# A transformer-style kernel in which the softmax of an attention block is finished in the step that follows its selection, with sums and reciprocals on GpSimd

## The chip, the cores and the metric

The kernel runs on one core of one Trainium2 chip. The metric is the device time of one execution in microseconds; the median of three runs is taken.

## The reference

Three layers follow one another. The first is attention that keeps, in every row of scores, the 32 largest only (batch 4, 8 heads, 576 tokens, 64 numbers per head):

```python
scores = scale * np.matmul(q, k.transpose(0, 1, 3, 2))
kth = np.partition(scores, -top_k, axis=-1)[..., -top_k:-top_k + 1]
scores = np.where(scores >= kth, scores, -1000000000.0)
scores = scores - np.max(scores, axis=-1, keepdims=True)
attn = np.exp(scores)
attn = attn / (np.sum(attn, axis=-1, keepdims=True) + 1e-09)
x = np.matmul(attn, v)
```

The second is a dense layer over 2304 tokens of width 512: softplus(x @ w_in) @ w_out, with 2048 hidden numbers. The third sends each token to the best of 8 experts, relu(x @ w1[e]) @ w2[e] with 1024 hidden numbers, times its gate.

## The kernel before

**Blocks.** The attention is cut into 72 blocks (BLOCKS). A block has 128 rows of two heads, so its scores are two tiles t = 0, 1 of 128 x 576. Rows 0 to 511 of a batch give four row groups of four head pairs each; the last 64 rows of two batches are taken together in "ends" blocks.

**Steps.** Every engine runs its own program, written out by hand as a loop over steps i = -1 to 73 (TAIL = 74); semaphores join the five programs. There is no planner: the order of the calls in each engine's loop is the schedule. Block n is selected on VectorE while step n runs, masked and exponentiated in step n+1, and in step n+2 it is normalised, transposed and multiplied with v. From step 10 (MLP_AT) on each step also does an eighth of the dense layer for a group of 256 tokens (unit u of group g): "up" in step i, "down" of the unit before. Group 0 needs the attention of blocks 0 to 7. The operations, with their lines in the profile:

- TensorE: scores (L575, eight products, in "ends" blocks sixteen), which writes the banks that scores_out empties; turn_probs (L589 and L592, nine transposes), which waits for pr_ready of each half; times_v (L614, 20 products, in "ends" blocks 40), which waits for probs_out; up (L644 to L646, 24 products); down (L663 to L665, 12 products); in some steps the turning of tokens (L676) and the logits (L686). The scores of block i+3 are made in step i (scores_at, AHEAD = 3), at its start; in the first step of a group they stand amid "up", before the product that needs the last block's x.
- ScalarE: scores_out (L887, L890), cut_off (L898, the first half of a mask), exponentials (L905), normalise (L911), probs_out (L918), x_out (L924), rectify (L932, L933), logarithm (L938, L941), h_high (L949), split_wo (L955), split_wi (L961), down_out (L970).
- VectorE: the selection, in four rounds of eight maxima for each tile (maxima L1158, strike L1164); reciprocals (L1172 the sum of two numbers for the first blocks, L1175 the reciprocal).
- GpSimd: biases (L1502, L1504), x_split_up (L1512, L1514), denominators (L1521, the sum, from block 9 on), mask (L1529 after a cut_off; L1533 and L1536 without one, a longer form), softplus (L1541), h_low (L1547), low_wo (L1552), low_wi (L1558).
- SyncE's queue: the loads, and the stores of split pieces of w_out (L464), which are read back in every group (L472).

Weights are split into a high and a low part (split_wo, low_wo, split_wi, low_wi) in steps 1 to 10, a piece in each step. cuts(n) says which tiles of block n are masked with ScalarE's help: both before block FREE = 8, tile 0 only afterwards. The scores stand in a ring of five buffers; top in a ring of three; pr, bias, eps, den and rden in two buffers. After step 73 come the last group of the dense layer and then the experts, in an order of their own.

In a step from 10 on the order on ScalarE is

```python
h_high(i-1); x_out(i-3); cut_off(i-1); scores_out(i+3)
normalise(i-2, 0); normalise(i-2, 1); rectify(i)
probs_out(i-2); turn_out / logits_out; logarithm(i)
exponentials(i-1, 0); exponentials(i-1, 1); down_out
```

and on GpSimd x_split_up(i-3), h_low(i-1), mask(i-1), low_wi, softplus(i), biases(i), denominators(i-1). VectorE's reciprocals(n-2) stand in the second round of block n. Before step 10 they stand behind the selection of the next block, so block n is normalised once block n+1 is selected.

## Time and profile before

| | before |
|---|---|
| median of 3 runs | 1057.04 us (1056.1 to 1057.84) |
| profiled execution | 1057.04 us, of it 1054.8 us span |
| TensorE (PE) busy | 992.9 us, 94% |
| VectorE (DVE) busy | 817.3 us, 77% |
| ScalarE (ACT) busy | 727.6 us, 69% |
| GpSimd (POOL) busy | 711.9 us, 67% |
| chain that ended last | PE 80%, DVE 8%, POOL 4%, ACT 3% |

The profile is one execution. A busy TensorE is not one at its peak: its products overlap, and their ends are modelled. The shares are means over the span; the attention and dense layer together run to about 742 us, the experts after that, and there only TensorE is full. A row of the view in order of time has the start, the duration of the group (both in us), the engine, the line, the operation, what it writes and reads, how many, and in brackets the idle time before it with what ended it. PE are the products, PEld the weight loads.

### The profile page before, as it was taken

Reading aid. Unit: us, or ns where it says so; the run is one execution under the profiler, and the core shown is the slowest. Engines: PE = TensorE matmul, PEld = TensorE weight load, DVE = VectorE, ACT = ScalarE, POOL = GpSimd, SP = SyncE. Lnnn points to the kernel's source line nnn. Section 1 sums busy time; section 2 is a strip of 40 time slices with the busy share of each in tenths; the row PEclk is TensorE's granted clock in tenths of the full one; section 3 lists DMA queues with packets and bytes.
Section 4 is the critical chain, followed back from the end, with each engine's and each line's share of the span. In section 5 each row is a group of like instructions: output and inputs, shape, how many; then the busy total and the mean of one; then the engine's idle time right before and its main releaser. Section 6 shows DMA issues by size and latency. Waiting matters only on the chain.

```text
span 1054.8 us, 21596 instructions
## 1 busy us (share of the span) xinstructions
PE 992.9 (94%) x6878; PEld 806.3 (76%) x6879; DVE 817.3 (77%) x1744; ACT 727.6 (69%) x1390; POOL 711.9 (67%) x831
## 2 busy tenths in 40 slices
PE   5565899999999999999999999999999999999996
PEld 2343687788788788788788888887887788888875
DVE  7999999999999999999999999994345622222261
ACT  3888898988998998998888999998554111111140
POOL 2688898889899899899888899899351311111101
PEclk9996899999999999999999999999999999999999
DMA  9723253343344343324434333333481421111100
GB/s 311 257 91 127 112 171 121 128 143 121 114 153 165 114 157 121 124 98 144 169 119 155 117 120 102 121 121 121 156 331 54 165 96 52 40 40 40 40 20 20
DMA packets 43391, 130.99 MB, mean 124 GB/s; under 512 B 4320, under 2 KB 18656, under 8 KB 33056
## 3 DMA queue, kind: packets, MB, share of 16 engines
q1 hardware_dynamic: 40256, 120.09, 32.5%
q0 software_dynamic: 3040, 9.70, 2.7%
q8 instruction: 51, 0.84, 0.3%
q14 instruction: 44, 0.36, 0.1%
HBM read 111.95 MB, written 18.09 MB: 123 GB/s over the span
## 4 chain that ended last, share of the span: by engine, by line
PE 80%; DVE 8%; POOL 4%; ACT 3%; issue 3%; DMA 1%; SPq 1%; ACTq 0%; DVEq 0%; POOLq 0%
PE psum L614 8%; PE psum L575 7%; PE psum L644 7%; PE psum L737 6%; PE psum L739 6%; PE psum L738 6%; PE psum L646 6%; PE psum L645 6%; PE psum L663 6%; PE psum L665 6%; PE psum L664 6%; PE psum L589 5%; DVE top L1158 3%; DVE work L1164 3%; PE psum L769 2%
## 5 line engine op out<-in xcount | busy, mean ns | idle before, releaser
L1158 DVE MAX8 top<-work 128x8 f32<-128x576 f32 x432 | 305.4, 752 | 0.0
L1164 DVE MATCH_REPLACE8 work<-top,work 128x576 f32<-128x576 f32 x288 | 212.6, 749 | 0.0
L644 PE MATMUL psum<-x_parts,wi_hi 128*128 128x256 f32 x576 | 171.1, 297 | 0.0
L645 PE MATMUL psum<-x_parts,wi_hi 128*128 128x256 f32 x576 | 162.9, 283 | 0.0
L646 PE MATMUL psum<-x_parts,wi_lo 128*128 128x256 f32 x576 | 162.7, 283 | 0.0
L614 PE MATMUL psum<-prT,vtok 128*64 128x128 f32 (+3 forms) x1600 | 117.1, 287 | 15.2 <-ACT prT L918 15.2
L614 PEld LDWEIGHTS psum<-prT,vtok 128*64 128x64 f32 (+1 forms) x1600 | 85.5, 144 | 54.2 <-issue 41.2
L575 PE MATMUL psum<-kT,qT 64*128 64x512 f32 (+3 forms) x640 | 113.0, 480 | 11.5 <-DMA qT<-in_q 4.4
L1638 POOL DMA_INDIRECT out<-ys,dst_now x19 | 19.2, 1012 | 152.6 <-DVE ys L1360 150.7
L663 PE MATMUL psum<-wo_ring,h_hi 128*128 x288 | 119.1, 414 | 1.0 <-POOL h_lo L1547 0.9
L1541 POOL TENSOR_TENSOR hs<-hs,ab 128x512 f32<-128x512 f32 x72 | 93.7, 1301 | 32.7 <-ACT ab L941 32.5
L644 PEld LDWEIGHTS psum<-x_parts,wi_hi 128*128 128x128 f32 x576 | 109.9, 191 | 6.8 <-issue 2.4
L905 ACT ACTIVATE pr<-pr,bias 128x576 f32<-128x576 f32 x144 | 110.0, 766 | 6.7 <-POOL pr L1536 3.7
L665 PE MATMUL psum<-wo_ring,h_lo 128*128 x288 | 113.1, 393 | 0.0
L664 PE MATMUL psum<-wo_ring,h_hi 128*128 x288 | 112.7, 391 | 0.0
L645 PEld LDWEIGHTS psum<-x_parts,wi_hi 128*128 128x128 f32 x576 | 110.1, 191 | 0.2
L646 PEld LDWEIGHTS psum<-x_parts,wi_lo 128*128 128x128 f32 x576 | 110.1, 191 | 0.0
L911 ACT ACTIVATE pr<-pr,rden 128x576 f32<-128x576 f32 x144 | 104.4, 784 | 8.0 <-DVE rden L1175 8.0
L575 PEld LDWEIGHTS psum<-kT,qT 64*128 64x128 f32 (+1 forms) x640 | 57.5, 195 | 68.1 <-issue 59.4
L589 PE MATMUL psum<-ident,pr 128*128 128x128 f32 x576 | 81.3, 284 | 22.3 <-ACT sc L890 16.7
L1547 POOL TENSOR_TENSOR h_lo<-hs,h_hi 128x512 fp32r<-128x512 f32 x72 | 93.1, 1293 | 5.9 <-ACT h_hi L949 5.9
L589 PEld LDWEIGHTS psum<-ident,pr 128*128 128x128 f32 x576 | 66.6, 145 | 27.9 <-issue 17.6
(215 smaller groups left out, 2353.1 us busy)
## 6 DMA issues: line engine op xcount, KB each, us to landing
wo_ring<-wo_parts SPq DMA_DIRECT2D x72, 1024.0 KB, 4.8
wo_parts<-wo_ring SPq DMA_DIRECT2D x8, 1024.0 KB, 3.8
kT<-in_k SPq DMA_DIRECT2D x16, 288.0 KB, 3.4
qT<-in_q SPq DMA_DIRECT2D x16, 288.0 KB, 3.9
vtok<-in_v SPq DMA_DIRECT2D x16, 256.0 KB, 2.9
wo_raw<-in_moe_w_out SPq DMA_DIRECT2D x1, 4096.0 KB, 14.1
wi_raw<-in_moe_w_in SPq DMA_DIRECT2D x4, 1024.0 KB, 14.4
x_rows<-x2tok SPq DMA_DIRECT2D x16, 256.0 KB, 2.4
```

Of the source, the lines that this page charges most:

```text
L575: mm = nc.tensor.matmul(to[rows, :], qT[h * HD:(h + 1) * HD, p, cols], kT[h * HD:(h + 1) * HD, p, keys], start=True, stop=True)
L589: mm = nc.tensor.transpose(transit[:, j // 3, j % 3 * P:(j % 3 + 1) * P], pr_of(n)[:, first_key(t) + c * P:first_key(t) + (c + 1) * P], id ...
L614: mm = nc.tensor.matmul(x_raw_at[h * HD:(h + 1) * HD, cols], vtok[rows, p, c, h * HD:(h + 1) * HD], probs, start=(c == 0), stop=(c == FULL))
L644: nc.tensor.matmul(ps[:, part, :], wi_hi[:, u, kk, f], hi, start=first, stop=False)
L645: nc.tensor.matmul(ps[:, part, :], wi_hi[:, u, kk, f], lo, start=False, stop=False)
L646: mm = nc.tensor.matmul(ps[:, part, :], wi_lo[:, u, kk, f], hi, start=False, stop=last)
L663: nc.tensor.matmul(psum[:, 6 + a, :], high, hi, start=(f == 0), stop=False)
L664: nc.tensor.matmul(psum[:, 6 + a, :], high, lo, start=False, stop=False)
L665: mm = nc.tensor.matmul(psum[:, 6 + a, :], low, hi, start=False, stop=(f == KF - 1))
L905: nc.scalar.activation(pr[:, n % 2 * 2 + t, :], pr[:, n % 2 * 2 + t, :], ACT.Exp, bias=bias[:, n % 2, 0, t:t + 1], scale=1.0, accum_out=ep ...
L1158: nc.vector.max(top[:, at, 8 * r:8 * r + 8], sc_of(n)[:, t, :] if r == 0 else work[:, t, :]).then_inc(topk_step, 1)
L1164: nc.vector.match_replace(work[:, t, :], top[:, at, 8 * r - 8:8 * r], sc_of(n)[:, t, :] if r == 1 else work[:, t, :], TAKEN).then_inc(topk ...
```

## The change

- On ScalarE, GpSimd and TensorE the calls of a step stand in a new order. Before step 10 ScalarE does probs_out, cut_off, split_wo, the exponentials, x_out (now of block i-2), scores_out and then normalise of block i-1, the one exponentiated just before. TensorE turns and multiplies block i-2 ahead of the scores.
- From step 10 on ScalarE does the exponentials of block i-2 at the start of the step, with x_out between the two, then scores_out, h_high, normalise, rectify, probs_out, cut_off, logarithm. GpSimd does biases(i-1), mask(i-1), softplus(i), x_split_up(i-2), denominators(i-1), h_low(i).
- VectorE no longer computes sums and reciprocals; denominators on GpSimd does, for every block: the sum, then a power with exponent -1 of two numbers per partition.
- Scores are made two blocks ahead from step 10 on, and none in step 9. FREE is 9, so both tiles of block 8 are cut with ScalarE's help.
- The load of w_out is issued in two halves with a semaphore each, and split_wo waits for the half that it reads.

The diff:

```diff
--- before.py
+++ after.py
@@ -89,7 +89,7 @@
             LOGITS[up_step(g) + UNITS + 2 + 2 * a] = 2 * g + a
 
 
-    FREE = MLP_AT - 2
+    FREE = MLP_AT - 1
 
     def cuts(n):
         return (0, 1) if n < FREE else (0,)
@@ -153,6 +153,7 @@
         ident = sb("ident", [P, P])
         wg = sb("wg", [P, KD, E])
         slot_no = sb("slot_no", [P, 2], I32)
+        inverse = sb("inverse", [P, 2])
         lg = sb("lg", [P, NT, E])
         eps = sb("eps", [P, 2, 2, 2])
 
@@ -284,7 +285,8 @@
         dst_now = sb("dst_now", [P, 1], I32)
         slot_gate = sb("slot_gate", [P, COLS])
 
-        wi_loaded, wo_loaded, wg_loaded = sem("wi_loaded"), sem("wo_loaded"), sem("wg_loaded")
+        wi_loaded, wg_loaded = sem("wi_loaded"), sem("wg_loaded")
+        wo_loaded = [sem("wo_loaded_0"), sem("wo_loaded_1")]
         wi_hi_ready, wi_split = sem("wi_hi_ready"), sem("wi_split")
         wo_hi_ready, wo_split = sem("wo_hi_ready"), sem("wo_split")
         wo_stored = [sem("wo_stored_0"), sem("wo_stored_1")]
@@ -300,6 +302,7 @@
         xs_split, e_h_split = sem("xs_split"), sem("e_h_split")
         gathered = [sem(f"gathered_{i}") for i in range(XS)]
         ident_step, consts = sem("ident_step"), sem("consts")
+        inverse_ready = sem("inverse_ready")
         scores_ready, scores_copied = sem("scores_ready"), sem("scores_copied")
         half_block, ends_copied = sem("half_block"), sem("ends_copied")
         topk_step, mask_step, masked = sem("topk_step"), sem("mask_step"), sem("masked")
@@ -329,13 +332,17 @@
 
 
 
-        AHEAD = 3
+
+        RING = 5
 
         def scores_at(i):
-            return i + 1 if i <= 0 else i + AHEAD
+            return i + 1 if i <= 0 else i + 3 if i < MLP_AT - 1 else i + 2 if i >= MLP_AT else BLOCKS
+
+        def scores_made(i):
+            return min(i + 4, MLP_AT + 2) if i < MLP_AT else min(i + 3, BLOCKS)
 
         def sc_of(n):
-            m = n % (AHEAD + 2)
+            m = n % RING
             return sc[:, 2 * m:2 * m + 2, :] if m < 3 else sc_more[:, 2 * m - 6:2 * m - 4, :]
 
         def is_block(n):
@@ -453,7 +460,10 @@
                 load_qk(0, p)
             for p in range(PAIRS):
                 load_v(0, p)
-            sp.dma_start(wo_raw[:], w_out.rearrange("(k p) n -> p k n", p=P)).then_inc(wo_loaded, 16)
+            for half in range(2):
+                at = slice(half * KF // 2, (half + 1) * KF // 2)
+                sp.dma_start(wo_raw[:, at, :], w_out.rearrange("(k p) n -> p k n", p=P)[:, at, :]
+                             ).then_inc(wo_loaded[half], 16)
             for kk in range(KD):
                 sp.dma_start(wi_raw[:, :, kk, :], w_in[kk * P:(kk + 1) * P, :].rearrange(
                     "p (u f) -> p u f", u=UNITS)).then_inc(wi_loaded, 16)
@@ -577,11 +587,11 @@
                                                   start=True, stop=True)
                 mm.then_inc(scores_ready, 1)
 
-            def turn_probs(n):
+            def turn_probs(n, made):
                 if n:
                     pe.wait_ge(transit_copied, n)
                     pe.wait_ge(x_copied, n)
-                pe.wait_ge(scores_copied, 2 * min(scores_at(n + 2) + 1, BLOCKS))
+                pe.wait_ge(scores_copied, 2 * made)
                 for t in range(2):
                     pe.wait_ge(pr_ready, 2 * n + t + 1)
                     for c in range(FULL):
@@ -797,16 +807,26 @@
             for i in range(-1, TAIL):
                 late = is_block(i - 2)
                 n = scores_at(i)
+                if i < MLP_AT:
+                    if late:
+                        turn_probs(i - 2, scores_made(i - 1))
+                        times_v(i - 2)
+                    if is_block(n):
+                        scores(n, max(i - 1, 0))
+                    if i == 0:
+                        scores(n + 1, 0)
+                        scores(n + 2, 0)
+                    continue
 
                 amid = {}
                 if up_at(i) and up_at(i)[1] == 0 and is_block(n):
-                    amid[0, k_last(up_at(i)[0])] = lambda: scores(n, max(i - 2, 0))
+                    amid[0, k_last(up_at(i)[0])] = lambda: scores(n, i - 2)
                 elif is_block(n):
-                    scores(n, max(i - 2, 0))
+                    scores(n, i - 2)
                 if up_at(i):
                     up(*up_at(i), amid)
                 if late:
-                    turn_probs(i - 2)
+                    turn_probs(i - 2, scores_made(i))
                 if i in TURNS:
                     turn_tokens(*TURNS[i], 0)
                 if i in LOGITS:
@@ -816,9 +836,6 @@
                         down(*down_at(i), part)
                 if late:
                     times_v(i - 2)
-                if i == 0:
-                    scores(n + 1, 0)
-                    scores(n + 2, 0)
 
             def last_down(u):
                 for part in range(2):
@@ -880,8 +897,8 @@
         def _(act):
             def scores_out(n):
                 act.wait_ge(scores_ready, n + 1)
-                if n >= AHEAD + 2:
-                    act.wait_ge(masked, 2 * (n - AHEAD - 2) + 2)
+                if n >= RING:
+                    act.wait_ge(masked, 2 * (n - RING) + 2)
                 to = sc_of(n)
                 to = to.rearrange("p t k -> p (t k)")
                 nc.scalar.mul(to[:, FULL * P:FULL * P + P].rearrange("p (t k) -> p t k", t=2), ends, SCALE
@@ -949,7 +966,7 @@
                 nc.scalar.copy(h_hi[:, n % 2], hs[:, n % 2]).then_inc(h_high_ready, 1)
 
             def split_wo(u):
-                act.wait_ge(wo_loaded, 16)
+                act.wait_ge(wo_loaded[u // (UNITS // 2)], 16)
                 if u >= 2:
                     act.wait_ge(wo_stored[u % 2], 16 * (u // 2))
                 nc.scalar.copy(wo_ring[:, u % 2, 0].bitcast(F32R), wo_raw[:, 2 * u:2 * u + 2, :]
@@ -1038,52 +1055,59 @@
                 now, late = is_block(i - 1), is_block(i - 2)
                 if i < MLP_AT:
                     if late:
-                        normalise(i - 2, 0)
-                        normalise(i - 2, 1)
-                    if is_block(i - 3):
-                        x_out(i - 3)
+                        probs_out(i - 2)
                     if now:
                         for t in cuts(i - 1):
                             cut_off(i - 1, t)
-                    scores_out(scores_at(i))
                     if wo_unit(i) is not None:
                         split_wo(wo_unit(i))
+
                     if now:
                         exponentials(i - 1, 0)
+                    if late and i == MLP_AT - 1:
+                        x_out(i - 2)
+                    if now:
                         exponentials(i - 1, 1)
-                    if late:
-                        probs_out(i - 2)
-                    if wi_unit(i) is not None:
-                        split_wi(wi_unit(i))
+                    if late and i < MLP_AT - 1:
+                        x_out(i - 2)
+                    if is_block(scores_at(i)):
+                        scores_out(scores_at(i))
                     if i == 0:
                         scores_out(scores_at(i) + 1)
                         scores_out(scores_at(i) + 2)
+                    if now:
+                        normalise(i - 1, 0)
+                        normalise(i - 1, 1)
+                    if wi_unit(i) is not None:
+                        split_wi(wi_unit(i))
                     continue
+                behind = late and i > MLP_AT
+                if behind:
+                    exponentials(i - 2, 0)
+                if is_block(i - 3) and i > MLP_AT:
+                    x_out(i - 3)
+                if behind:
+                    exponentials(i - 2, 1)
+                if is_block(scores_at(i)):
+                    scores_out(scores_at(i))
                 if up_at(i - 1):
                     h_high(*up_at(i - 1))
-                if is_block(i - 3):
-                    x_out(i - 3)
-                if now:
-                    for t in cuts(i - 1):
-                        cut_off(i - 1, t)
-                if is_block(scores_at(i)):
-                    scores_out(scores_at(i))
-                if late:
+                if behind:
                     normalise(i - 2, 0)
                     normalise(i - 2, 1)
                 if up_at(i):
                     rectify(*up_at(i))
                 if late:
                     probs_out(i - 2)
+                if now:
+                    for t in cuts(i - 1):
+                        cut_off(i - 1, t)
                 if i in TURNS:
                     turn_out(TURNS[i][1], 0)
                 if i in LOGITS:
                     logits_out(LOGITS[i], 1)
                 if up_at(i):
                     logarithm(*up_at(i))
-                if now:
-                    exponentials(i - 1, 0)
-                    exponentials(i - 1, 1)
                 if down_at(i) and down_at(i)[1] == UNITS - 1:
                     down_out(down_at(i)[0])
 
@@ -1165,15 +1189,6 @@
                                         sc_of(n)[:, t, :] if r == 1 else work[:, t, :], TAKEN
                                         ).then_inc(topk_step, 1)
 
-
-            def reciprocals(n):
-                if n < MLP_AT - 1:
-                    dve.wait_ge(exp_ready, 2 * n + 2)
-                    nc.vector.tensor_reduce(den[:, n % 2, :], eps[:, n % 2], AX.X, ALU.add
-                                            ).then_inc(den_step, 1)
-                dve.wait_ge(den_step, n + 1)
-                nc.vector.reciprocal(rden[:, n % 2, :], den[:, n % 2, :]).then_inc(rden_ready, 1)
-
             for ring_credit in (dst_step, e_y_raw):
                 dve.sem_inc(ring_credit, CREDIT)
             for ring_credit in (w1_loaded[1], w2_loaded[1]):
@@ -1183,14 +1198,8 @@
                     for t in range(2):
                         if r:
                             strike(n, t, r)
-                    if r == 1 and n > MLP_AT:
-                        reciprocals(n - 2)
                     for t in range(2):
                         maxima(n, t, r)
-                if 0 < n < MLP_AT:
-                    reciprocals(n - 1)
-            reciprocals(BLOCKS - 2)
-            reciprocals(BLOCKS - 1)
 
             def low(rank, first, end, hi_ready, done):
                 par = rank % 2
@@ -1517,9 +1526,12 @@
             def denominators(n):
                 pool.wait_ge(exp_ready, 2 * n + 2)
                 if n >= 2:
-                    pool.wait_ge(rden_ready, n - 1)
+                    pool.wait_ge(pr_ready, 2 * n - 2)
                 nc.gpsimd.tensor_tensor(den[:, n % 2, :], eps[:, n % 2, :, 0], eps[:, n % 2, :, 1],
                                         ALU.add).then_inc(den_step, 1)
+                pool.wait_ge(den_step, n + 1)
+                nc.gpsimd.tensor_tensor(rden[:, n % 2, :], den[:, n % 2, :], inverse[:], ALU.pow
+                                        ).then_inc(rden_ready, 1)
 
             def mask(n, t):
                 at = n % 3 * 2 + t
@@ -1565,6 +1577,7 @@
             nc.gpsimd.iota(slot_no[:], pattern=[[1, 2]], base=0, channel_multiplier=0
                            ).then_inc(consts, 1)
             nc.gpsimd.memset(eps[:], 1e-9).then_inc(consts, 1)
+            nc.gpsimd.memset(inverse[:], -1.0).then_inc(inverse_ready, 1)
             nc.gpsimd.memset(ones[:], 1.0).then_inc(ident_step, 1)
             pool.wait_ge(ident_step, 2)
 
@@ -1587,28 +1600,34 @@
             pool.wait_ge(ident_step, 3 + BATCH // 2)
             nc.gpsimd.memset(scan_mask[:, :, 0:1], 0.0).then_inc(consts, 1)
 
+            pool.wait_ge(inverse_ready, 1)
             for i in range(TAIL):
-                if i >= MLP_AT and is_block(i - 3):
+                now = is_block(i - 1)
+                if now:
+                    biases(i - 1)
+                if i < MLP_AT and is_block(i - 3):
                     x_split_up(i - 3)
-                if up_at(i - 1):
-                    h_low(*up_at(i - 1))
-                if is_block(i - 1):
+                if now:
                     for t in tiles_of(i - 1):
                         mask(i - 1, t)
-                if i < MLP_AT and is_block(i - 3):
-                    x_split_up(i - 3)
+                if i < MLP_AT:
+                    if i == MLP_AT - 1:
+                        x_split_up(i - 2)
+                    if wo_unit(i) is not None:
+                        low_wo(wo_unit(i))
+                    if now:
+                        denominators(i - 1)
+                else:
+                    if up_at(i):
+                        softplus(*up_at(i))
+                    if is_block(i - 2):
+                        x_split_up(i - 2)
+                    if now:
+                        denominators(i - 1)
+                    if up_at(i):
+                        h_low(*up_at(i))
                 if wi_unit(i - 1) is not None:
                     low_wi(wi_unit(i - 1))
-                if wo_unit(i) is not None:
-                    low_wo(wo_unit(i))
-                if up_at(i):
-                    softplus(*up_at(i))
-                if is_block(i):
-                    biases(i)
-                if is_block(i - 1) and i - 1 >= MLP_AT - 1:
-                    denominators(i - 1)
-            x_split_up(BLOCKS - 1)
-            h_low(LASTG - 1, UNITS - 1)
             for u in range(5):
                 softplus(LASTG, u)
                 h_low(LASTG, u)
```

## Rows read from the trace of the kernel before

**Rows 1.** Busy time by stretch: start:end, length, busy us of each engine, PEclk, DMA

```profile
88.00:98.00 10.00, 6.00 (x41) 3.97 (x41) 9.97 (x24) 8.47 (x15) 8.66 (x9) 0.67 0.26 106
...
300.00:400.00 100.00, 99.87 (x776) 82.36 (x773) 98.86 (x214) 90.68 (x181) 90.13 (x102) 1.00 0.45 152
```

**Rows 2.** In order of time, TensorE, the steps before the first up

```profile
53.92 1.94 PE L589 MATMUL psum<-ident,pr 128*128 128x128 f32 x8 [1.56 <-ACT sc L890]
...
93.31 1.06 PE L589 MATMUL psum<-ident,pr 128*128 128x128 f32 x8 [1.91 <-ACT sc L890]
...
96.57 2.60 PE L614 MATMUL psum<-prT,vtok 128*64 128x128 f32 x20 [2.09 <-ACT prT L918]
...
109.85 0.58 PE L644 MATMUL psum<-x_parts,wi_hi 128*128 128x256 f32 x1
```

**Rows 3.** In order of time, TensorE: a plain step, a group's first, the last steps

```profile
259.46 1.30 PE L575 MATMUL psum<-kT,qT 64*128 64x512 f32 x8
...
263.66 1.03 PE L589 MATMUL psum<-ident,pr 128*128 128x128 f32 x8
...
268.91 0.39 PE L644 MATMUL psum<-x_parts,wi_hi 128*128 128x256 f32 x1
...
278.96 1.30 PE L575 MATMUL psum<-kT,qT 64*128 64x512 f32 x8
...
696.04 1.46 PE L614 MATMUL psum<-prT,vtok 128*64 128x128 f32 x20
...
740.70 1.46 PE L614 MATMUL psum<-prT,vtok 128*64 128x128 f32 x20
```

**Rows 4.** In order of time, ScalarE, the same two steps

```profile
259.13 0.61 ACT L949 CAST h_hi<-hs 128x512 fp32r<-128x512 f32 x1
...
260.81 0.28 ACT L887 ACTIVATE sc_more<-psum 128x128 f32<-128x128 f32 x1 [0.23 <-PE psum L575]
...
261.94 1.45 ACT L911 ACTIVATE pr<-pr,rden 128x576 f32<-128x576 f32 x2
...
271.51 0.28 ACT L887 ACTIVATE sc_more<-psum 128x128 f32<-128x128 f32 x1 [1.48 <-PE psum L575]
```

**Rows 5.** In order of time, GpSimd, the same steps

```profile
259.65 0.19 POOL L1521 TENSOR_TENSOR den<-eps 128x2 f32<-128x2 f32 x1
...
269.12 0.19 POOL L1521 TENSOR_TENSOR den<-eps 128x2 f32<-128x2 f32 x1
...
269.80 0.46 POOL L1514 TENSOR_TENSOR x_parts<-xraw,x_parts 128x128 fp32r<-128x128 f32 x1
```

**Rows 6.** The chain that ended last, in order of time

```profile
148.85 1.95 PE psum L575 x16
...
248.70 1.39 PE psum L614 x20
...
327.52 1.39 PE psum L614 x20
```

**Rows 7.** In order of time, VectorE

```profile
7.70 1.42 DVE L1158 MAX8 top<-sc 128x8 f32<-128x576 f32 x2 [7.55 <-ACT sc L890]
...
17.35 1.41 DVE L1158 MAX8 top<-sc 128x8 f32<-128x576 f32 x2
...
98.71 0.17 DVE L1175 RECIPROCAL rden<-den 128x2 f32<-128x2 f32 x1
```

**Rows 8.** In order of time, ScalarE and GpSimd, the steps before the first up

```profile
38.72 1.04 ACT L961 CAST wi_hi<-wi_raw 128x1024 fp32r<-128x1024 f32 x1 [1.82 <-DMA wi_raw<-in_moe_w_in]
...
46.18 1.12 ACT L918 COPY prT<-psum 128x1152 f32<-128x1152 f32 x1
...
90.48 1.44 ACT L898 ACTIVATE pr<-sc,bias 128x576 f32<-128x576 f32 x2
...
91.34 2.78 POOL L1529 TENSOR_TENSOR pr<-sc,pr 128x576 f32<-128x576 f32 x2 [1.10 <-ACT pr L898]
...
97.16 2.37 POOL L1552 TENSOR_TENSOR wo_ring<-wo_raw,wo_ring 128x1024 fp32r<-128x1024 f32 x1
```

## Prediction

> **What bounds the kernel now.** I read the page first, then busy time by stretch, then each engine in order of time inside one step. TensorE is busy 94% of the span by the page, and in its middle 99.87 of 100 us; the idle time lies ahead of 120 us: it was busy 6.0 of 10 us from 88 to 98 us, at a granted clock of 0.67 [rows 1]. So two numbers set the time: when the first "up" product starts (109.85 us [rows 2]), and what a step costs from there on. I call T the moment at which TensorE is through with times_v of the step before, and s a step's wait at turn_probs.
>
> In a plain step TensorE starts at 259.46 with the scores, turns the probabilities at 263.66 (T+4.20) and is back at 268.91: 9.45 us, without a gap [rows 3]. The normalised halves come from ScalarE: it sees the scores at T+1.35, and normalises from 261.94 = T+2.48 [rows 4]. The second half is wanted four transposes of 0.11 us after the first, at T+4.64; with the 1.45 us of both halves and some 0.11 us to release, normalise may begin as late as T+3.08. The slack is 0.60 us. In the first step of a group of eight, where the scores stand amid "up", ScalarE sees them at 271.51 = T+2.60 and normalises 1.13 us on as before, from T+3.73 [rows 4]. The turning waits for it: this step takes 278.96 - 268.91 = 10.05 us [rows 3]. The scores' second fill costs some 0.1; the rest is s = 0.47, so the latest free start of normalise is T+3.26 there. GpSimd is nearly full: its additions of denominators stand at 259.65 and 269.12, 9.47 us apart with no gap [rows 5], while a group of eight steps takes TensorE 327.52 - 248.70 = 78.82 us, 9.85 each [rows 6]. It catches up in the longer steps (turned tokens and logits).
>
> **The change, part by part.**
> VectorE loses a reciprocal of 0.17 us per block, early with the sum ahead of it; a block without them took 17.35 - 7.70 = 9.65 us [rows 7]. Block 7 is then selected at 7.70 + 8 x 9.65 = 84.9 us; before, block 8, the next, was through ahead of the reciprocal at 98.71, so block 7 near 88.7. This is worth nothing by itself, as the next part shows; VectorE is never the late one afterwards.
>
> Start. Softmax of block n now ends in the step that follows its selection, so a loop closes through one step: cut to mask 0.86 (90.48 to 91.34), two masks 2.73, low_wo 2.45 (2.37 at 97.16 and 0.08 more) [rows 8]; sum 0.28 (0.19 and 0.09 until a dependent operation starts [rows 5]) and power 0.29, if it lasts 0.20; on ScalarE, where the next operation starts some 0.1 ahead of an end, two normalises 1.34 (1.45 [rows 4]), split_wi 0.95 (1.04) and probs_out 1.02 (1.12 [rows 8]). Sum 9.9 us. Turning eight blocks took 1.94 us at 53.92 and 1.06 at 93.31 [rows 2]; with the ninth, 2.15 at half clock and 1.2 at full. At half clock probs_out waits for it, and the loop takes 10.8 us. Either is above VectorE's 9.65, so the loop bounds. It starts when split_wi(0) is free of its load, 38.72 us [rows 8]; probs_out of step 3 ends near 41.0, normalise of block 2 starts at 47.6, and five loops later (three slow, two between) that of block 7 at 99.7. Its turning, probs_out and times_v (2.60 us at half clock, at 96.57 [rows 2]) end at 105.9. So the first "up" starts at 105.9 instead of 109.85: -3.9 us. With all loops at full clock it is 103.0, with all slow 107.6. The wo_raw load cut in two lets ScalarE split sooner, but the wi load at 38.72 comes after it and holds anyway: 0. SyncE's queue stores each split piece after low_wo, now later in its step, and it is wanted two steps on: 0.
>
> First steps after it. Block 9 is the first with the long mask, and GpSimd still has low_wi(6) and low_wi(7), 2.37 us each, as the low_wo at 97.16 [rows 8]. I follow it: step 10 takes 10.0 us (T 115.9), step 11 9.45 and s = 0.6, step 12 9.45 and s = 2.8, for low_wi(7) delays block 10's masks, step 13 some 10.2. TensorE is at 148.4 where it was at 148.85 [rows 6]: of 3.9 us only 0.4 is left.
>
> Steady steps. Two things are new. First, h_high (0.61 us at 259.13 [rows 4], 0.52 until the next can start) stands between scores_out and normalise: normalise from T+3.00, just inside T+3.08; in the first step of a group from T+4.25, and s grows from 0.47 to 0.99. Second, the order on GpSimd is now h_low, biases, masks, softplus, x_split, sum, power, and normalise waits for its end, while h_low may not begin before h_high has ended, at T+3.17. Its period is 9.45 + 0.28 for the power = 9.73 us. After h_low at T+3.17 the reciprocals are there at T+12.91, in a plain step T'+3.46: s = 0.38, then 0.31. After the first step of a group h_low starts at T+4.42, and the next step waits 0.5. Even a power for nothing leaves a loop over the last mask, exponential, scores_out and h_high of 9.51 to 9.68 us. The scores a block less far ahead cost VectorE nothing, for it starts a block more than a step before GpSimd wants it, and the next batch's q and k loads keep their two blocks' distance from their use on SyncE's queue: 0. The long steps reset the lag and give nothing back, since h_low waits for h_high in them. One group: 0.52 + 0.51 + 0.38 + 0.31 = +1.7 us. Over steps 14 to 68: seven first steps, +3.6; six second ones (in one the two-batch piece hides it), +2.9; five pairs of plain steps, +3.4.
>
> Power. All 72 lie in the loop, and no row shows one. The same two elements added take 0.19 us, a two-operand pass over 128 elements 0.46 [rows 5]. I take 0.20, nearest to the addition (same shape and engine); 0.46 makes the period 9.99 us, longer than TensorE's mean step, and by the same walk the total +21 instead of +13. Below 0.19 saves at most 0.05 x 60 = 3. The Trainium skill says to leave elementwise work to VectorE, GpSimd being about 2x slower (GPSIMD Engine Reference, section 4.1): twice VectorE's reciprocal would be 0.33 us, and the sum some 4 us more.
>
> End. In the last five steps there are no scores to hide behind: TensorE's times_v lie 740.70 - 696.04 = 44.7 us apart over them [rows 3], and TensorE's own work would be some 42: GpSimd's 9.45 already set the pace. With 9.73, no initial slack, and one more block of scores left to this part (fewer are ahead), I get 48.5: +3.8. After them the order is the old one: 0.
>
> Sum: -0.4 + 3.6 + 2.9 + 3.4 + 3.8 = +13.3 us on the profiled execution, 1057.04 us (span 1054.8 and 2.2 around it), which is also the median: 1070.
>
> **The rivals.**
> Faster: the lead at the start is kept. Mechanism: turn_probs tolerates the later normalise, because the releases are shorter than I count. It decides at T+3.08 in plain steps and at a GpSimd period of 9.45. Then 3.9 to 6.8 us are won: 1050 to 1053, and 1055 with the first-of-group waits. For it: the margin in plain steps is hundredths, and TensorE shows no gap in the middle; against: the old first step of a group already waits by this very path.
> The waits in the steady steps and at the end come at half of the 13.7 us, and the start keeps part of its 3.9: 1056 to 1062, part of it no change.
> The power is slow: 1078 for 0.46 us, more above it; it decides where the period passes TensorE's 9.85. For and against: GpSimd's smallest operations cost mostly their start, so only a library routine would be long; nothing in the trace excludes it.
> The change does not reach the start: if the split loop runs slow throughout and the masks of block 9 come still later, first "up" at 107.6 to 110: 1072 to 1074.
>
> **How the numbers follow.** My forecast (1064 to 1074) has 0.39, the slow power 0.14, the start that is not reached 0.06, the half losses 0.16 (half of it within 0.2%), the kept lead 0.25. A measurement of this kernel tells some 0.2% (2.1 us) from no change. So faster 0.25, same 0.08, slower 0.67. The range takes in most of the kept lead and the power at 0.46: 1051 to 1079.
>
> **What would show it.** The first "up" between 103 and 108 us; the power's own duration (0.2 us); GpSimd's sums 9.7 us apart in plain steps; first steps of a group at 10.5 instead of 10.05 us and the second at 10.4 instead of 9.9; waits of turn_probs for normalise, and of ScalarE's normalise for the power; VectorE without reciprocals and idle. I am wrong if a group of eight steps still takes 78.8 us, or if the "up" product starts before 100 us.

## The result and the profile after

The changed kernel takes **1086.84 us** (median of 4 runs, 1085.68 to 1089.29) against 1056.89 of the kernel before on the same chip: ratio 1.0286, 95% interval 1.0266 to 1.0306. It is slower by 30 us, where 13 were forecast, and above the range. Its profiled execution took 1087.35 us, 1085.6 of it span.

The page of the changed kernel: the head, and the chain that ended last.

```profile
span 1085.6 us, 21609 instructions
...
PE 1005.6 (93%) x6878; PEld 808.6 (74%) x6879; DVE 814.3 (75%) x1663; ACT 738.3 (68%) x1391; POOL 759.2 (70%) x912
...
POOL 43%; PE 27%; DVE 15%; issue 10%; ACT 3%; SPq 1%; DMA 1%; ACTq 0%; DVEq 0%; POOLq 0%
```

GpSimd's busy share rose only from 67 to 70%, yet its part of the chain went from 4 to 43%, and TensorE's fell from 80 to 27%. The share of busy time hides this, the chain shows it.

The power (instructions that write or read rden, changed kernel), and the waits by total:

```profile
L1533 POOL TENSOR_TENSOR rden<-den,inverse x72: 708/722/731, 25.9 to 766.9; 128x2 f32<-128x2 f32 x72
```

```profile
PE psum L599 <- ACT pr L928: 41.9, 35, 5.5
DVE top L1182 <- POOL pr L1541: 35.2, 59, 2.5
ACT pr L922 <- POOL pr L1548: 24.4, 48, 2.2
POOL h_lo L1559 <- ACT h_hi L966: 20.9, 33, 1.7
ACT pr L928 <- POOL rden L1533: 20.5, 40, 1.1
```

The first row has minimum, median and maximum in ns: the power of two elements per partition lasts **0.72 us**, where I had taken 0.20 and an upper end of 0.46. The waits (total us, times, longest) show the path that I had named: TensorE's turning waits for the normalised halves, and ScalarE's normalise for the power.

Two steps of the changed kernel in order of time, GpSimd:

```profile
363.17 0.20 POOL L1530 TENSOR_TENSOR den<-eps 128x2 f32<-128x2 f32 x1
363.44 0.72 POOL L1533 TENSOR_TENSOR rden<-den,inverse 128x2 f32<-128x2 f32 x1
364.90 1.28 POOL L1559 TENSOR_TENSOR h_lo<-hs,h_hi 128x512 fp32r<-128x512 f32 x1 [0.73 <-ACT h_hi L966]
...
373.98 0.20 POOL L1530 TENSOR_TENSOR den<-eps 128x2 f32<-128x2 f32 x1
374.25 0.72 POOL L1533 TENSOR_TENSOR rden<-den,inverse 128x2 f32<-128x2 f32 x1
374.94 1.28 POOL L1559 TENSOR_TENSOR h_lo<-hs,h_hi 128x512 fp32r<-128x512 f32 x1
```

From h_low at 364.90 to the next at 374.94 GpSimd shows no gap: 10.04 us, where [rows 5] had 9.47 between two sums, and more than TensorE's mean of 9.85. Of these 0.69 are the power, from its start to that of the next operation, and some 0.1 is its wait for the sum. The same steps on ScalarE and TensorE:

```profile
364.19 0.63 ACT L966 CAST h_hi<-hs 128x512 fp32r<-128x512 f32 x1
364.70 1.46 ACT L928 ACTIVATE pr<-pr,rden 128x576 f32<-128x576 f32 x2
...
375.00 0.78 ACT L928 ACTIVATE pr<-pr,rden 128x576 f32<-128x576 f32 x1 [0.41 <-POOL rden L1533]
```

```profile
360.45 0.39 PE L654 MATMUL psum<-x_parts,wi_hi 128*128 128x256 f32 x1
...
361.71 1.30 PE L585 MATMUL psum<-kT,qT 64*128 64x512 f32 x8
...
365.64 1.23 PE L599 MATMUL psum<-ident,pr 128*128 128x128 f32 x8 [0.31 <-ACT pr L928]
```

T is 360.45 here, the first step of a group. ScalarE reaches normalise at T+4.25, behind h_high, exactly where the prediction put it. In the next step h_high is done at 374.60, and normalise waits for the power until 375.00.

At the start, in order of time on GpSimd and ScalarE and then on TensorE:

```profile
89.45 2.35 POOL L1564 TENSOR_TENSOR wo_ring<-wo_raw,wo_ring 128x1024 fp32r<-128x1024 f32 x1
91.76 0.20 POOL L1530 TENSOR_TENSOR den<-eps 128x2 f32<-128x2 f32 x1
92.03 0.71 POOL L1533 TENSOR_TENSOR rden<-den,inverse 128x2 f32<-128x2 f32 x1
```

```profile
92.78 1.44 ACT L928 ACTIVATE pr<-pr,rden 128x576 f32<-128x576 f32 x2 [0.54 <-POOL rden L1533]
```

```profile
96.70 2.60 PE L624 MATMUL psum<-prT,vtok 128*64 128x128 f32 x20 [1.21 <-ACT prT L935]
...
107.52 2.60 PE L624 MATMUL psum<-prT,vtok 128*64 128x128 f32 x20 [1.21 <-ACT prT L935]
110.05 0.58 PE L654 MATMUL psum<-x_parts,wi_hi 128*128 128x256 f32 x1
```

This is the loop of the prediction, link by link (masks, low_wo, sum, power, normalise), at 10.7 to 11.1 us a block. The first "up" starts at 110.05, against 109.85 [rows 2] and 105.9 predicted. VectorE keeps to 9.66 us a block meanwhile, as the two rows below show (order of time, VectorE, first maxima of blocks 0 and 1): it has lost the reciprocals, and nothing comes of it.

```profile
7.72 1.42 DVE L1182 MAX8 top<-sc 128x8 f32<-128x576 f32 x2 [7.58 <-ACT sc L907]
17.38 1.40 DVE L1182 MAX8 top<-sc 128x8 f32<-128x576 f32 x2
```

### The profile page after: what moved, and what is told of

It is laid out like the page before. It is cut to its first block, busy times and chain, and to the rows that moved or that the text cites. A ratio compares the mean times of both kernels' runs of the same rounds, so it can differ in the third digit from the quotient of the medians.

```text
span 1085.6 us, 21609 instructions
## 1 busy us (share of the span) xinstructions
PE 1005.6 (93%) x6878; PEld 808.6 (74%) x6879; DVE 814.3 (75%) x1663; ACT 738.3 (68%) x1391; POOL 759.2 (70%) x912
## 4 chain that ended last, share of the span: by engine, by line
POOL 43%; PE 27%; DVE 15%; issue 10%; ACT 3%; SPq 1%; DMA 1%; ACTq 0%; DVEq 0%; POOLq 0%
POOL pr L1545 13%; POOL pr L1541 9%; DVE top L1182 8%; POOL pr L1548 7%; PE psum L747 6%; PE psum L748 6%; PE psum L749 6%; DVE work L1188 6%; POOL hs L1553 3%; POOL h_lo L1559 3%; POOL rden L1533 2%; POOL wo_ring L1564 2%; PE psum L599 2%; PE psum L779 2%; POOL bias L1511 1%
## 5 line engine op out<-in xcount | busy, mean ns | idle before, releaser
L922 ACT ACTIVATE pr<-pr,bias 128x576 f32<-128x576 f32 x144 | 111.8, 776 | 40.4 <-POOL pr L1548 24.4
L599 PE MATMUL psum<-ident,pr 128*128 128x128 f32 x576 | 89.2, 293 | 43.7 <-ACT pr L928 41.9
L585 PE MATMUL psum<-kT,qT 64*128 64x512 f32 (+3 forms) x640 | 112.8, 479 | 10.1 <-DMA qT<-in_q 4.4
## 6 DMA issues: line engine op xcount, KB each, us to landing
wo_raw<-in_moe_w_out SPq DMA_DIRECT2D x2, 2048.0 KB, 12.2
```

The lines of the kernel that those rows point to most:

```text
L585: mm = nc.tensor.matmul(to[rows, :], qT[h * HD:(h + 1) * HD, p, cols], kT[h * HD:(h + 1) * HD, p, keys], start=True, stop=True)
L599: mm = nc.tensor.transpose(transit[:, j // 3, j % 3 * P:(j % 3 + 1) * P], pr_of(n)[:, first_key(t) + c * P:first_key(t) + (c + 1) * P], id ...
```

## The experiments

Two theories stood at the outset. **A**: the order costs about what the prediction said, and the rest is the power's 0.72 us. **B**: the order costs most of it by a path not counted, such as VectorE's wait for the masks (35.2 us above), and the power is beside the point. The measure is the start of times_v of one block in the profiled executions. What follows block 71 is 314.1 us in the kernel before and 312.8 to 313.2 us in every other kernel with all outputs, those with the old order included, so a difference at block 71 is about 1 us larger than that of the whole. Line numbers in the diffs are left out.

**1. A cheap operation in the power's place.**

```diff
-nc.gpsimd.tensor_tensor(rden[...], den[...], inverse[:], ALU.pow)
+nc.gpsimd.tensor_tensor(rden[...], den[...], inverse[:], ALU.mult)
```

> The changed kernel, with a multiplication by the same tile in place of GpSimd's power (so the probabilities are not divided by their sums; everything else is done). Theory A, the length of the power (0.72 us) in GpSimd's loop makes most of the loss: the multiplication takes about 0.2 us, GpSimd's h_low in plain steps stand 9.6 to 9.7 us apart instead of 10.05, and the time falls from 1087 to 1065 to 1071; what is left over 1057 is the order's. Theory B, the order (h_high ahead of normalise, h_low at the end, exponentials at the start) makes most of it whatever the operation costs: above 1080. Theory C, VectorE is late since scores and maxima wait for masks: unchanged, 1085 or more.

Measured: 1168.84 us in all. This kernel leaves out the division by the sums, so its results are others and so is its work in the experts (7058 TensorE products in all, 6878 before); only the part up to block 71 compares. There times_v starts at 750.9, against 740.7 before [rows 3] and 772.6 after. The multiplication:

```profile
L1533 POOL TENSOR_TENSOR rden<-den,inverse x72: 194/195/198, 26.3 to 745.8; 128x2 f32<-128x2 f32 x72
```

So 0.53 us less per block takes 21.7 of the 31.9 us away, for A; the first "up" came at 104.7.

**2. The power in the old order**, from block 9 on.

```diff
 def denominators(n):
+    pool.wait_ge(den_step, n + 1)
+    nc.gpsimd.tensor_tensor(rden[...], den[...], inverse[:], ALU.pow).then_inc(rden_ready, 1)
 def reciprocals(n):
+    if n >= MLP_AT - 1:
+        return
```

> The kernel before, with GpSimd's power in place of VectorE's reciprocal from block 9 on, and no other edit. Theory A: GpSimd's period grows from 9.43 to about 10.05 us, above TensorE's mean of 9.85, so 62 steps cost 0.2 us each and more at the end: 1070 to 1076. Theory B: the old order hides it, for GpSimd's wait does not reach turn_probs: 1057 to 1061.

Measured: 1067.92 us, ratio 1.0109 (1.0092 to 1.0126): +11.6 us, between the two theories and nearer to A. GpSimd's period became 10.1 us here too, and the group up to blocks 24 to 31 takes 80.75 us, eight of these periods. ScalarE's waits for the reciprocals hardly grew (9.6 us, 8.0 before): that GpSimd is full is enough.

**3. The new order only before step 10**, the old one from there.

```diff
-return i + 1 if i <= 0 else i + 3 if i < MLP_AT - 1 else i + 2 ...
+return i + 1 if i <= 0 else i + 3
+if r == 1 and n > MLP_AT:
+    reciprocals(n - 2)
...
```

> The new order, GpSimd's sums and powers and the halved load before step 10 only; from step 10 on the old order, with VectorE's reciprocals and the scores three blocks ahead. Theory A: the first up product starts at 110 to 113 us as in the changed kernel (110.0), against 109.85 before, for the loop through low_wo and the power takes 10.7 to 11.1 us; steps then cost as before: 1056 to 1060. Theory D, the new start costs the time: above 1065. Theory E, the new start does save a few us and the steady steps hide it: below 1054.

Measured: 1061.09 us, ratio 1.0044 (1.0027 to 1.0061), 1 us above theory A. With the power inside, the start alone costs some 4.7 us. From times_v of block 7 to that of block 8 this kernel takes 12.7 us and to that of block 9 13.5 more (steps 10 and 11), and in order of time GpSimd shows low_wi(6) and low_wi(7) between the masks:

```profile
113.39 2.38 POOL L1578 TENSOR_TENSOR wi_lo<-wi_raw,wi_hi 128x1024 fp32r<-128x1024 f32 x1
...
121.52 2.37 POOL L1578 TENSOR_TENSOR wi_lo<-wi_raw,wi_hi 128x1024 fp32r<-128x1024 f32 x1
```

**4. Four buffers for the maxima instead of three**, so that VectorE need not wait for the masks.

```diff
-top = phase("top", [P, 6, TOPK])
+top = phase("top", [P, 8, TOPK])
-if n >= 3: dve.wait_ge(masked, 2 * (n - 3) + 2)
+if n >= 4: dve.wait_ge(masked, 2 * (n - 4) + 2)
```

> The changed kernel with four buffers instead of three for the maxima (top), so that VectorE's first maxima of a block wait for the masks of the block four before instead of three. The profile shows 35 us of such waits. Theory A: VectorE has a block in hand, its waits only follow GpSimd: the waits go or move, the time stays within 1 us of 1087. Theory C, VectorE's late start delays biases and masks: 1075 or less.

Measured: 1088.02 us, ratio 1.0299 (1.0282 to 1.0316), as without it. The largest wait that had looked like a cause was the slack of an engine that is early: it moved to the scores.

**5. The order without the power**, a first try: VectorE takes the reciprocals back, at fixed places.

```diff
+if r == 3 and 0 < n < MLP_AT:     reciprocals(n - 1)
+if r == 1 and n > MLP_AT + 1:     reciprocals(n - 3)
-nc.gpsimd.tensor_tensor(rden[...], den[...], inverse[:], ALU.pow)
```

> The changed kernel with the power taken off GpSimd and VectorE's reciprocal back (in block n's fourth round for block n-1 up to block 8, in block n's second round for block n-3 from block 9 on); GpSimd keeps the sums. The output is the full one, so the whole time counts. Theory A, the power is the mis-sized term and the order costs the rest: GpSimd's period falls to 9.5 to 9.7 us, the last times_v ends 5 to 9 us after that of the kernel before instead of 32, the time is 1061 to 1066, first steps of a group still 10.57 us. Theory B, the order costs most: above 1075. Theory F, the order costs nothing: within 2 us of 1056.5.

Measured: **1087.1 us**, ratio 1.0287 (1.0272 to 1.0303), as slow as with the power, against A. The trace in order of time, GpSimd and VectorE:

```profile
349.60 0.20 POOL L1540 TENSOR_TENSOR den<-eps 128x2 f32<-128x2 f32 x1
...
359.39 0.20 POOL L1540 TENSOR_TENSOR den<-eps 128x2 f32<-128x2 f32 x1
```

```profile
350.50 0.15 DVE L1194 RECIPROCAL rden<-den 128x2 f32<-128x2 f32 x1
...
360.31 0.16 DVE L1194 RECIPROCAL rden<-den 128x2 f32<-128x2 f32 x1
```

```profile
132.89 1.44 ACT L928 ACTIVATE pr<-pr,rden 128x576 f32<-128x576 f32 x2 [11.21 <-DVE rden L1194]
```

A reciprocal of 0.16 us stands 0.7 us behind the end of its sum, behind VectorE's strikes of another block, which is as late as a power of 0.72; and block 9's stood in VectorE's block 12, and ScalarE waited 11.21 us for it. The run had put a new wait in the power's place (at block 11 it is already 12.8 us late, and 18.5 more come by block 66), so it does not decide between A and B. Run 9 repeats it without that.

**6. Run 5 with h_high behind normalise only outside the groups' first steps.** The diff gives h_high its old place ahead of the scores in those first steps.

```diff
+first = up_at(i) and up_at(i)[1] == 0
+if first and up_at(i - 1):
+    h_high(*up_at(i - 1))
-if up_at(i - 1):
+if not first and up_at(i - 1):
     h_high(*up_at(i - 1))
```

> As the run before, with h_high ahead of scores_out in the first step of each group only, where the scores come late. Theory A (in these steps normalise waits for h_high's 0.52 us, and GpSimd's h_low starts later by as much, which makes the next step wait too): first steps fall from 10.57 to about 10.05 us, the next ones by up to 0.5, in all 4 to 7 us less than the run before. Rival: the first step is bound by the turning and the down products, h_high is hidden: no change beyond 1 us.

Measured: 1082.34 us, ratio 1.0245 (1.0229 to 1.0261), 4.8 less than run 5, inside what A asked. The prediction's first-step term was 3.6 and part of the second's. Since run 5 has a wait of its own there, this supports the term and does not size it.

**7. Run 3 with low_wo behind the sum and the power.**

```diff
-if wo_unit(i) is not None: low_wo(wo_unit(i))
 if now: denominators(i - 1)
+if wo_unit(i) is not None: low_wo(wo_unit(i))
```

> The kernel of the early order alone (1061.1 us), with low_wo on GpSimd behind the sum and the power instead of ahead of them, before step 10. Theory A (low_wo's 2.45 us lies in the loop mask, low_wo, sum, power, normalise, turning, probs_out, cut): the blocks before step 10 go from 11.0 us apart to 9.9 to 10.3, where GpSimd's own sum of work bounds; times_v of block 7 starts at 101 to 104 instead of 107.9, and the time falls by 3 to 5 us. Rival (the start is bound by TensorE at half clock or by ScalarE's splits): unchanged within 1 us.

Measured: 1058.09 us, ratio 1.0016 (1.0006 to 1.0025), 3.0 less than run 3: low_wo was indeed a link of the start's loop. The blocks before step 10 stand 10.6 us apart, 11.0 in run 3, and not the 9.9 to 10.3 of theory A: of low_wo's 2.45 us only 0.4 came back, so another path is close behind it. No run tells which.

**8. Run 7 with VectorE's reciprocals for the first nine blocks**, so no power anywhere.

```diff
+if r == 3 and 0 < n < MLP_AT: reciprocals(n - 1)
 def denominators(n):
-    nc.gpsimd.tensor_tensor(rden[...], den[...], inverse[:], ALU.pow)
```

> As the run before, with VectorE's reciprocals for blocks 0 to 8 too (in the fourth round of the next block), so no power at all; from step 10 on everything is as in the kernel before. Theory A: the start is bound by VectorE's 9.82 us a block, times_v of block 7 starts at 97 to 101, but from step 11 on the old order needs block n selected by the start of step n+1, so only 2 to 4 us are kept: 1052.5 to 1055. If the lead is given back to the long masks and low_wi in steps 10 to 12, it is within 1 us of the kernel before.

Measured: **1052.37 us**, ratio 0.9962 (0.9948 to 0.9975), faster than both kernels. The first "up" (order of time, TensorE, this kernel):

```profile
106.48 0.58 PE L654 MATMUL psum<-x_parts,wi_hi 128*128 128x256 f32 x1
```

It starts 3.4 us earlier than at 109.85 [rows 2], and the time falls by 3.8. At times_v of block 7 the lead is 5.7 us, at block 11 2.3 and at block 71 3.0. So about half of the start's lead can be kept, if the new order ends at step 10. The power cost 5.7 us there, against run 7.

**9. The order without the power, the reciprocals met.** As run 5, but each reciprocal stands in VectorE's order where VectorE had got to when that block's sum ended in run 1 (14 instructions a block); due stands ahead of every maximum and strike.

```diff
+def due(m):
+    n = done[1]
+    if done[0] >= 14 * n + (LAG[n] if n < len(LAG) else 45):
+        reciprocals(n); done[1] += 1
+    done[0] += 1
```

> The changed kernel without the power, with all its outputs: VectorE takes the 72 reciprocals (0.16 us each) back, and each stands in VectorE's order where VectorE had got to at the end of that block's sum in the kernel with the cheap operation (14 instructions a block; block n's stands ahead of the instruction 14n + 45, and 14n + 27 to 14n + 44 for the first 19 blocks), where the kernel of the experiment on the order alone had put it up to 0.9 us behind the sum in steady steps and some 11 us behind at block 9. Theory A (the order costs what the prediction said, and its placing of the reciprocals made the earlier kernel late): times_v of block 71 at 750 to 753, and 1066 to 1071 us in all. Rival (the order itself costs +30, and the cheap operation hid it by the numbers it changed): times_v of block 71 above 765, and 1082 to 1088.

Measured: **1068.65 us**, ratio 1.0120 (1.0105 to 1.0136), +12.2 us; times_v of block 71 at 752.9, which is theory A's. GpSimd in order of time:

```profile
345.50 0.20 POOL L1549 TENSOR_TENSOR den<-eps 128x2 f32<-128x2 f32 x1
346.20 1.29 POOL L1575 TENSOR_TENSOR h_lo<-hs,h_hi 128x512 fp32r<-128x512 f32 x1 [0.51 <-ACT h_hi L966]
...
355.29 0.20 POOL L1549 TENSOR_TENSOR den<-eps 128x2 f32<-128x2 f32 x1
```

The steps here are 9.8 us apart with GpSimd idle in them, waiting for h_high (56.9 us in all, 67 times, against 5.9 before). So the order has a loop of its own. By the calls it runs over last mask, exponential, scores_out, h_high, h_low and masks; the wait for h_high is the part that the trace shows.

**10. Two powers.**

```diff
+nc.gpsimd.tensor_tensor(spare[...], den[...], inverse[:], ALU.pow)
 nc.gpsimd.tensor_tensor(rden[...], den[...], inverse[:], ALU.pow)
```

> The changed kernel with each block's power computed twice, the first result into a spare tile that nobody reads. Theory A (GpSimd's own chain of 10.05 us a block is the bound of the steps, and each 0.72 us of it is paid in every step): a chain of 10.77, +0.72 in each of about 61 steps from step 10 on and +0.6 in each of the first eight: 1087 + 44 to 50, so 1128 to 1138 us. Rival (something else sets the 10.05, the power is only near it): 1088 to 1100.

Measured: 1122.33 us, ratio 1.0633 (1.0615 to 1.0652): 35.5 us on top of the change, far from the rival's 1 to 13 and under the 41 to 51 that A had asked. In order of time on GpSimd:

```profile
369.71 0.72 POOL L1534 TENSOR_TENSOR spare<-den,inverse 128x2 f32<-128x2 f32 x1
370.40 0.69 POOL L1535 TENSOR_TENSOR rden<-den,inverse 128x2 f32<-128x2 f32 x1
...
380.39 0.72 POOL L1534 TENSOR_TENSOR spare<-den,inverse 128x2 f32<-128x2 f32 x1
```

The period is 10.68 us, 0.64 more than 10.04, and a group of eight steps takes 85.7 us, which is eight periods (85.4): GpSimd alone sets the pace. In the change a group took 82.1 where eight periods are 80.3, for TensorE's long steps still added to it. So a group pays 3.6 us for the second power and not 8 x 0.64 = 5.1. From block 11 to 66 that makes 23.8 us more than the change, where A had asked some 40; at the start it is 8.1, more than the 4.8 of A.

**11. The two halves of the load alone.**

```diff
-sp.dma_start(wo_raw[:], ...).then_inc(wo_loaded, 16)
+for half in range(2):
+    sp.dma_start(wo_raw[:, at, :], ...).then_inc(wo_loaded[half], 16)
```

> The kernel of before with only the load of the output weights cut into two halves with a semaphore each. Theory A (it is worth nothing, as predicted, and the gain of the early order with VectorE's reciprocal is the order's): 1055.5 to 1056.8 us. Rival (the gain came from the load): 1052 to 1054.

Measured: 1055.85 us, ratio 0.9996 (0.9987 to 1.0005): nothing, as predicted.

**12. The power by its width**, on numbers that nobody reads.

```diff
+for w in (2, 16, 128):
+    for op in (ALU.pow, ALU.mult):
+        nc.gpsimd.tensor_tensor(pr[:, 2 + at % 2, :w], pr[:, 0, :w], pr[:, 1, :w], op)
```

> The changed kernel with three powers and three multiplications of 2, 16 and 128 elements per partition ahead of GpSimd's loop, on numbers that nobody reads. If the power is dear by its elements (0.72 less 0.195 us over 2 elements is some 0.26 us each): 4.4 us for 16 and some 34 us for 128. If it is a fixed cost of some 0.5 us an instruction: 0.75 us for 16 and about 1 us for 128 (the multiplication 0.2 and 0.4 us). The total is not compared.

GpSimd's groups by line and shape; each row is one power and one multiplication (line, engine, operation, shapes, count, then total us and mean ns):

```profile
L1588 POOL TENSOR_TENSOR pr<-pr 128x128 f32<-128x128 f32 x2 | 21.2, 10615 | 0.2
L1588 POOL TENSOR_TENSOR pr<-pr 128x16 f32<-128x16 f32 x2 | 3.1, 1568 | 0.2
...
L1588 POOL TENSOR_TENSOR pr<-pr 128x2 f32<-128x2 f32 x2 | 0.9, 467 | 0.2
```

The single rows are 0.732, 2.916 and 20.774 us for the powers and 0.202, 0.219 and 0.456 for the multiplications. The power costs (20.774 - 2.916) / 112 = **0.16 us per element** of a partition and some 0.4 to begin with; neither of the two expectations, a fixed cost or 0.26 each, was right.

## Why the prediction was wrong

The times_v starts put the difference in its place (profiled executions, us more than before; "old order" is run 2):

```
                            predicted  run 1  run 9   after   run 10  old order
to block 11 (147.39)             -      -1.2   +1.1    +6.2   +14.3      +0.6
blocks 11 to 66 (548.65)         -      +8.5   +9.0   +19.5   +43.4      +8.6
blocks 66 to 71 (44.66)         +3.8    +2.9   +2.1    +6.2    +8.0      +3.0
at block 71 (740.70)           +13.3   +10.2  +12.2   +31.9   +65.6     +12.2
```

The lengths of a group's eight steps, up to blocks 24 to 31:

```
before  10.05  9.94 10.32  9.85 10.32  9.45  9.45  9.45   78.83
run 1   10.57 10.25 10.32  9.88 10.32  9.40  9.74  9.75   80.23
after   10.57 10.79 10.50  9.88 10.69  9.40 10.23 10.06   82.12
```

**The step that failed** is the term "Power": "I take 0.20, nearest to the addition (same shape and engine)". It measured 0.72 us, 3.6 times that, beyond the end of 0.46 which I had drawn from a two-operand pass over 128 elements. That end bounded size, not kind: no row before showed a power, and an operation of unknown kind is not bounded by rows of another kind. The rival "The power is slow: 1078 for 0.46 us, more above it" was the right mechanism, with 0.14 too small a chance, and with its "nothing in the trace excludes it" it should have moved the range's upper end. By the prediction's own price, 21 - 13.3 = 7.7 us for 0.26, the 0.72 would have given 13.3 + 15.4 = 28.7; 30 were measured. That this comes so close is partly luck. By the prediction's walk the period would be 9.45 + 0.28 + 0.52 = 10.25 us, and it is 10.04; in return the power cost 5 us in the start, which stands under "Start" below.

The Trainium skill's rule (GPSIMD Engine Reference, section 4.1: elementwise work to VectorE, GpSimd being about 2x slower) pointed the right way. The section gives that factor for additions, multiplications and maxima of two inputs, and the prediction carried it over to a power: 0.72 against the 0.16 us of VectorE's reciprocal of the same 128x2 elements is 4.5.

**Start: -0.4.** The loop held in the link that was tested (run 7, low_wo) and nearly in its length: with the multiplication of 0.195 us it took 10.1 to 10.2 us, and the first "up" came at 104.7, for 105.9. With 0.72 each round is some 0.5 to 0.9 longer, and 110.05 less 104.71 makes 5.3 us over the rounds: the lead was gone. That low_wi(6), low_wi(7) and the long mask eat 3.5 us behind it came about in run 1 (of a lead of 5.1 at block 7, 107.33 less 102.18, 1.2 is left at block 11); run 3 shows the two low_wi in the way. The split into slow and fast rounds by TensorE's clock did not show. Runs 5 and 6 are the same program before step 10; from 40 to 100 us the mean granted clock was 1.00 in the profiled run 5 and 0.50 to 0.59 in run 6, and the blocks stood 10.5 and 10.2 us apart. The two are 2.6 us apart at block 7, so a smaller difference between two single traces of the start shows nothing.

**First steps of groups: 3.6.** 10.57 predicted, 10.57 measured in run 1 and in the changed kernel. **Second steps: 2.9**, 0.4 to 0.5 each: 10.25 in run 1 (+0.31), 10.79 after, where the power adds its share. **Pairs of plain steps: 3.4**: 9.83 and 9.76 predicted, 9.74 and 9.75 in run 1, 10.23 and 10.06 after. The sum of the three, 9.9, stands against 8.5 and 9.0 in runs 1 and 9 from block 11 to 66. **End: 3.8** for 2.9 and 2.1, and 6.2 after.

**GpSimd's period.** "Its period is 9.45 + 0.28 = 9.73" came out (9.74), for another reason. Its own work without the power is 10.04 - 0.69 - 0.12 = 9.23 us, the 0.12 for the wait on the sum (the power starts 0.27 us after it, h_low in run 9 0.15); the shortest periods of run 9, at its end, are 9.22 and 9.25. The 9.45 of the prediction was TensorE's plain step, which GpSimd followed with waits too short for the view. In runs 1 and 9 GpSimd waits for h_high in nearly every step, so what sets 9.74 is most likely the loop that the prediction named and put at 9.51 to 9.68. In steady steps the power's first part goes into that wait, and it is GpSimd's own 10.04 that counts after it. (9.23 + 0.12 + 0.4 = 9.75: by this estimate a power of up to some 0.4 us would have been mostly hidden there, which no run tried.)

**VectorE** "never the late one" held (run 4), and so did the load (run 11). **The rival of the kept lead** fell by the steady steps: run 8 keeps it only by going back to the old order at step 10.

**How the 30 us split.** The order alone +12.2 (run 9), the power in the order the rest, 18. In the old order the same power costs 11.6 from block 9 on. At block 71 the two make 24.4 of the 31.9 us in the table. Of the missing 7.5, 4.4 lie ahead of block 11, where the changed kernel has the power in every round and run 2 has it only from block 9 on; 1.9 lie between blocks 11 and 66 and 1.1 behind, and no run explains these.

What stays open: run 9 is 2.4 us behind run 1 at block 11. That can be the placing of its first reciprocals or no more than the difference of two traces (2.6 us in runs 5 and 6). In the first case the order itself costs some 10 us and the power some 20; it was not tried.

## What to carry to other kernels

An operation that the trace does not show needs a bound of its own kind: the same shape and engine do not bound a power by an addition, and where it lies in a loop whose engine is full, the upper end has to be several times the nearest row (here it was 3.6 times). Before moving small work to an engine, look at how much of its period is free in the stage that counts and not at its share of the span: GpSimd's 67% before were 90% from 300 to 700 us, and the 70% of the changed kernel were 93% there. When an experiment moves work back to an engine with an order of its own, place it where that engine is when the input is ready, or the run measures the placing (runs 5 and 9, 18 us apart).

## What the runs showed of the hardware

I had not expected GpSimd's power to cost by the element: 0.73 us for 2 elements per partition, 2.92 for 16 and 20.8 for 128, against 0.20, 0.22 and 0.46 for a multiplication (run 12); VectorE's reciprocal of two takes 0.16. So the prediction's remark that GpSimd's smallest operations cost mostly their start holds for the multiplication; the power of two elements has some 0.3 of its 0.72 us in the elements. Nor had I expected that a second power right behind the first is nearly as dear (0.69 against 0.72 in run 10), so a first-time cost is not what makes it long.
